# Three-stage attention and mixer kernel: ScalarE moves both accumulator halves, and the orders of the seam, the tail terms and the last sums change

## The chip, the cores and the metric

The kernel runs on one core of a Trainium2 chip. The core has engines with queues of their own: TensorE (PE in the profile, its weight loads PEld), VectorE (DVE), ScalarE (ACT), GpSimd (POOL) and SyncE (SP, which here only issues DMAs). Each engine executes its instructions in the order in which they were written; engines wait for one another through semaphores. The metric is the device time of one execution in microseconds (us), lower is better.

## The reference

Three blocks follow one another: attention with pooled queries, a gated block with spatial mixing, and a token and channel mixer. All tensors are float32.

```python
q_pool = q.reshape(B, H, S // 2, 2, D).mean(axis=3)            # B 4, H 8, S 1152, D 64
scores = 1.0 / np.sqrt(D) * np.matmul(q_pool, k.transpose(0, 1, 3, 2))
attn = softmax(scores)                                          # 576 x 1152 for each head
x = heads_side_by_side(np.matmul(attn, v))                      # [4, 576, 512]

h = gelu_tanh(x @ w_in)                                         # [4, 576, 1024]
u, v = h[..., :512], h[..., 512:]
v_n = (v - mean(v)) / np.sqrt(var(v) + 1e-06) * g_ln
v_s = np.einsum('ts,bsd->btd', w_sg, v_n) + b_sg[None, :, None]
x = x + (u * v_s) @ w_out

h = np.maximum(x.transpose(0, 2, 1) @ w_tok1, 0.0) @ w_tok2     # 576 -> 256 -> 576
u = x + h.transpose(0, 2, 1)
out = u + np.maximum(u @ w_ch1, 0.0) @ w_ch2                    # 512 -> 1536 -> 512
```

## The kernel before

Every float32 product outside the value products and transposes is made of three: each operand is split into a rounded high part and a low rest (high by ScalarE or GpSimd, low by VectorE or GpSimd), and `three` (L785) issues high x high, low x high and high x low. `stacked` (L791) does with two products for the fifth token tile, which has 64 rows: its high and low parts lie one above the other in `n_tail` and `xn_tail`, those of two batches in one pair of tiles, even batch and odd batch.

The activations stay in SBUF as `xT` [128, 16 slabs, 576], transposed; a slab is a pair of heads, four slabs are a batch.

Attention runs over 16 pairs of heads i, each in 9 steps s (four query tiles of the first head, one tile with the last 64 queries of both heads at `TAIL_STEP` 4, four tiles of the second head). In a step TensorE transposes the probabilities of four steps ago (`transpose_p`, L661), multiplies some of the transposed probabilities of the pair before with v (`values`, L732, in the bank `ACC_BANK`, first half of the queries on partitions 0 to 63, second half on 64 to 127), and makes scores in banks 0 to 3 (`scores`, L698). VectorE takes the scores out with their maximum (`take`, L1247), ScalarE does the exponential (`exps`, L1043), VectorE the reciprocal of the sum (`recip`, L1258), GpSimd the scaling (`norm`, L570), and ScalarE and VectorE move half of the transposed probabilities each (`evac_p`). The value products of a pair's first head end in step 3 of the next pair, those of its second head in step 8; then the accumulator is moved to `xT`: the first 288 queries by ScalarE (`acc_copy`, L1057), the other 288 by VectorE (`acc_copy`, L1271). The first `values` of the next head waits for both. Step 8 has its value products first, the other steps the transposes. The order on each engine is written out by `step` (L750, L1062, L1276).

The seam comes next. TensorE makes the first two v tiles of batch 0 (`v_tile`, L800) between the value products, then the rest of the value products, then `gated` (L884), which follows the list `GELU`: for batch 0 u 0, v 2, v 3, v 4, u 1, u 2, u 3. v tile 2 uses the bank of v tile 0 and waits for its gelu. A gelu takes a square and a tanh of ScalarE (L1097, L1108) and two operations of VectorE (`poly`, L1322, and `gelu`, L1331), which for a v tile is followed by its statistics; GpSimd raises the variance to -1/2 (`norm_rstd`, L630), VectorE normalises, and the result is split into `n_h` and `n_l` or `n_tail`. The orders at the seam stand in L1154 to L1172 for ScalarE and in L1433 to L1451 for VectorE; `sg_hi` and `sg_lo` split w_sg, `xe_hi_of` and `xe_lo_of` split the tails of x for v tile 4. GpSimd splits w_out behind its wait for the last accumulator copy (L625), and SP loads b_row and g_col behind the same (L503).

The spatial products are pairs of banks e = 4 to 7 (`pair`, L841), with five terms for each of two halves of the tokens, one half after the other; for e = 4 the fifth term waits for `n_tail`.

In the last block `to_tokens` (L820) transposes x, `h1_product` (L921) makes the first token product, in which batch b uses its rows of `xn_tail`; `tokens_lo` (L1376) fills both halves of it and signals once. `token_mix` (L945) makes four u products in banks 4 to 7, and VectorE adds each to `xT` (`u_added`). In the last batch VectorE does four subtractions (`u_lo_of(0)`) ahead of these four sums. Then come four chunks of 512 tokens and one of the four tails (`chunk`, L1017), all five with f products in banks 0 to 3 and y products in banks 4 to 7.

## Time and profile before

| | us |
|---|---|
| median of 3 runs | 1028.44 (1027.86 to 1028.56) |
| the profiled execution | 1028.56 |
| its span, first to last instruction | 1026.8 |
| TensorE busy | 992.4 |
| VectorE busy | 585.4 |
| ScalarE busy | 446.2 |
| GpSimd busy | 382.3 |

The first v tile starts at 440.6 us of the span, the tokens of the last block at 652, the chunks at 727. The granted TensorE clock is 0.995 of the full one in the mean. Matmul ends in the profile are modelled and overlap the next start, so steps are best read from start to start. In a timeline a number in brackets is the idle time of that engine before the row, with what ended it; rows of one kind that follow closely are merged, with their count.

### The profile page before, as it was taken

To read this page: it belongs to the slowest core of one execution; us is meant where nothing else is said; L and a number is where in the kernel's file an instruction comes from. 1 tells how busy PE (TensorE), PEld (TensorE's weight loads), DVE (VectorE), ACT (ScalarE), POOL (GpSimd) and SP (SyncE) were. 2 spreads that over 40 slices of the span, in tenths; PEclk is the share of its full clock that TensorE was granted. 3 is DMA by queue.
4 is the path that set the end of the run, shared out by engine and by line. 5 is a ranking of instruction groups with operands and counts; after the bars stand their busy time and mean duration, and the time that the engine had idled before them with its cause. 6 is when DMAs were issued, how large, how long until landed. Compare 5 with 4: busy or idle time off the path is not lost.

```text
span 1026.8 us, 23142 instructions
## 1 busy us (share of the span) xinstructions
PE 992.4 (97%) x8980; PEld 816.3 (80%) x8980; DVE 585.4 (57%) x1157; ACT 446.2 (43%) x846; POOL 382.3 (37%) x296
## 2 busy tenths in 40 slices
PE   7799999999999999889999999999999999999998
PEld 7577777777777767659999999988888888888898
DVE  5687877777778887778585867554312113131121
ACT  3677777777777777645151523131111111011111
POOL 3777777777777777631000102287000000000000
PEclk9999999999999999999999999999999999999999
DMA  5644444444444433320000000143000001001010
GB/s 164 183 117 116 115 115 115 115 115 115 115 115 115 115 89 78 112 79 1 1 2 1 2 1 1 55 115 102 1 1 15 26 0 41 0 0 41 0 41 22
DMA packets 34026, 65.54 MB, mean 64 GB/s; under 512 B 6208, under 2 KB 14784, under 8 KB 33984
## 3 DMA queue, kind: packets, MB, share of 16 engines
q1 hardware_dynamic: 33824, 64.34, 22.1%
q10 hardware_dynamic: 160, 0.59, 0.2%
q8 instruction: 32, 0.52, 0.2%
q14 instruction: 10, 0.08, 0.0%
HBM read 42.93 MB, written 4.72 MB: 46 GB/s over the span
## 4 chain that ended last, share of the span: by engine, by line
PE 83%; DVE 7%; issue 5%; DMA 2%; POOL 1%; ACT 1%; SPq 0%; DVEq 0%; ACTq 0%; POOLq 0%
PE ps L787 17%; PE ps L788 16%; PE ps L789 16%; PE ps L745 12%; PE ps L728 10%; PE ps L679 6%; DVE prob L1254 2%; PE ps L714 1%; DVE pT L1269 1%; PE ps L715 1%; PE ps L716 1%; PE ps L836 1%; DMA q_two<-in_q 1%; POOL prob L575 1%; DVE gbuf L1326 1%
## 5 line engine op out<-in xcount | busy, mean ns | idle before, releaser
L1254 DVE TENSOR_SCALAR_CACHE_REDUCE prob<-ps 128x1152 f32<-128x1152 f32 x144 | 195.5, 1358 | 74.2 <-PE ps L728 55.8
L575 POOL TENSOR_SCALAR prob<-prob,rsum 128x1152 f32<-128x1152 f32 x144 | 177.6, 1233 | 114.4 <-DVE rsum L1263 114.0
L1047 ACT ACTIVATE prob<-prob,nmax 128x1152 f32<-128x1152 f32 x144 | 181.1, 1258 | 16.8 <-DVE prob L1254 10.0
L745 PE MATMUL ps<-pT,v_sb 128*64 128x288 f32 x1152 | 171.5, 420 | 2.0
L1493 DVE SCALAR_TENSOR_TENSOR f_l<-ps,f_h 128x512 fp32r<-128x512 f32 (+1 forms) x60 | 38.3, 638 | 222.7 <-ACT f_h L1204 222.7
L1034 ACT ACTIVATE pT<-ps 128x512 f32<-128x512 f32 (+1 forms) x288 | 109.5, 432 | 97.6 <-PE ps L679 97.5
L1204 ACT ACTIVATE f_h<-ps 128x512 fp32r<-128x512 f32 (+1 forms) x60 | 33.3, 555 | 256.3 <-PE ps L789 256.3
L728 PE MATMUL ps<-k_over,q_over 64*128 64x288 f32 x744 | 131.2, 309 | 4.0 <-DVE prob L1254 4.0
L728 PEld LDWEIGHTS ps<-k_over,q_over 64*128 64x128 f32 x744 | 102.4, 185 | 24.2 <-DVE prob L1254 22.7
L679 PEld LDWEIGHTS ps<-ident,prob 64*128 64x128 f32 x2592 | 99.6, 139 | 20.4 <-issue 20.4
L679 PE MATMUL ps<-ident,prob 64*128 64x64 f32 x2592 | 106.9, 224 | 6.1 <-POOL prob L575 3.0
L745 PEld LDWEIGHTS ps<-pT,v_sb 128*64 128x64 f32 x1152 | 71.2, 136 | 44.1 <-issue 8.7
L1269 DVE COPY pT<-ps 128x512 f32<-128x512 f32 x144 | 98.9, 687 | 10.0 <-PE ps L679 10.0
L788 PE MATMUL ps<-u_l,c_h 128*128 128x512 f32 (+1 forms) x240 | 88.3, 368 | 0.0
L787 PE MATMUL ps<-u_h,c_h 128*128 128x512 f32 (+1 forms) x240 | 88.3, 368 | 0.0
L789 PE MATMUL ps<-u_h,c_l 128*128 128x512 f32 (+1 forms) x240 | 88.3, 368 | 0.0
L787 PE MATMUL ps<-f_h,c_h 128*128 128x512 f32 (+1 forms) x240 | 88.3, 368 | 0.0
L788 PE MATMUL ps<-f_l,c_h 128*128 128x512 f32 (+1 forms) x240 | 88.3, 368 | 0.0
L789 PE MATMUL ps<-f_h,c_l 128*128 128x512 f32 (+1 forms) x240 | 88.3, 368 | 0.0
L728 PE MATMUL ps<-kh,qh 64*128 64x288 f32 x248 | 85.1, 343 | 2.1 <-DMA k_over<-kl 2.1
L634 POOL TENSOR_TENSOR rstd<-var_e,minus_half 128x1 f32<-128x1 f32 x18 | 13.7, 761 | 162.5 <-DVE var_e L1351 162.5
L728 PE MATMUL ps<-kl,qh 64*128 64x288 f32 x248 | 72.4, 292 | 0.0
(153 smaller groups left out, 2144.0 us busy)
## 6 DMA issues: line engine op xcount, KB each, us to landing
q_raw<-in_q SPq DMA_DIRECT2D x16, 640.0 KB, 4.9
k_raw<-in_k SPq DMA_DIRECT2D x16, 576.0 KB, 3.9
v_sb<-in_v SPq DMA_DIRECT2D x32, 288.0 KB, 2.9
k_over<-kh SPq DMA_DIRECT2D x31, 144.0 KB, 2.5
k_over<-kl SPq DMA_DIRECT2D x31, 144.0 KB, 2.6
out_x<-xT SPq DMA_DIRECT2D x4, 1024.0 KB, 4.2
q_over<-qh SPq DMA_DIRECT2D x31, 128.0 KB, 2.3
q_over<-ql SPq DMA_DIRECT2D x31, 128.0 KB, 2.4
```

Of the source, the lines that this page charges most:

```text
L575: g.tensor_scalar(sl, sl, rsum[:, s:s + 1], 0.0, ALU.mult, ALU.add).then_inc(norm_done, 1)
L679: ins = te.transpose(dst, prob[half, PROB_BUF[s], j * P:(j + 1) * P], ident[half, half])
L728: ins = te.matmul(ps[:, 2 * m + t, 0:CK], w, x, start=(term == 0), stop=(term == 2))
L745: ins = te.matmul(ps[PH * c:PH * c + PH, ACC_BANK, 0:n], v_sb[:, a, j, :], pT[:, a, j, c * n:c * n + n], start=(j == 0), stop=(j == KB - 1))
L787: te.matmul(acc, wh, xh, start=start, stop=False)
L788: te.matmul(acc, wh, xl, start=False, stop=False)
L789: return te.matmul(acc, wl, xh, start=False, stop=stop)
L1034: return sc.activation(o, i_, ACT.Copy)
L1047: sc.activation(sl, sl, ACT.Exp, scale=-1.0, bias=nmax[:, s:s + 1], accum_out=esum[:, s:s + 1]).then_inc(exp_done, 1)
L1254: ve.tensor_scalar(prob[:, PROB_BUF[s], :].rearrange("p (c n) -> p c n", c=SCORE_BANKS), ps[:, 0:SCORE_BANKS, 0:CK], -SCALE, BIG, ALU.mult ...
L1269: ve.tensor_copy(pT_of(s, 1), trans(1)).then_inc(pT_by_dve, 1)
L1493: ve.scalar_tensor_tensor(out=f_l[:, f % F_N, 0:n], in0=ps[:, f % F_N, 0:n], scalar=0.0, in1=f_h[:, f % F_N, 0:n].bitcast(F32), op0=ALU.ma ...
```

## The change

In attention ScalarE moves both halves of the accumulator in two instructions, and VectorE moves none; one semaphore, `acc_moved`, counts four for a pair. At the seam tanh and gelu of v tiles 0 and 1 move ahead of the last accumulator copy, w_sg's last subtraction and the x tails behind it, and GpSimd's first two `norm_rstd` ahead of the w_out split. For e = 4 the fifth terms of both halves follow the first four terms of both. The odd half of `xn_tail` gets a semaphore of its own, `xn_odd`. In the last batch the u products use banks 4, 6, 0 and 2, VectorE does two of the four subtractions ahead of the first sum and two ahead of the fourth, and the first chunk is written out of the loop with waits for the sums.

```diff
@@ -376,6 +376,11 @@
+        def u_bank(b, c):
+            return (4, 6, 0, 2)[c] if b == B - 1 else 4 + 2 * (c % 2)
@@ -500,8 +505,7 @@
-            sp.wait_ge(acc_by_act, 2 * NP)
-            sp.wait_ge(acc_by_dve, 2 * NP)
+            sp.wait_ge(acc_moved, 4 * NP)
             sp.dma_start(b_row[:, :], b_sg.partition_broadcast(P)).then_inc(small_in, 16)
@@ -622,19 +626,21 @@
-            pool.wait_ge(acc_by_act, 2 * NP)
-            pool.wait_ge(acc_by_dve, 2 * NP)
-            for u in range(U_WO, U_T1):
-                split_w(u)
+            norm_rstd(0, 0)
+            norm_rstd(0, 1)
+            pool.wait_ge(acc_moved, 4 * NP)
+            for u in range(U_WO, U_T1):
+                split_w(u)
             for b in range(B):
-                for m in range(tiles(b)):
+                for m in range(2 if b == 0 else 0, tiles(b)):
                     norm_rstd(b, m)
@@ -733,8 +739,7 @@
                     if not (isinstance(i, int) and i + a == 0):
-                        pe.wait_ge(acc_by_act, at(i, 2, a))
-                        pe.wait_ge(acc_by_dve, at(i, 2, a))
+                        pe.wait_ge(acc_moved, at(i, 4, 2 * a))
                     last = TAIL_STEP if a == 0 else NS - 1
@@ -801,6 +806,9 @@
                     pe.wait_ge(xe_split, b // 2 + 1)
+                    if b == 0:
+                        pe.wait_ge(acc_moved, 4 * NP)
                     pe.wait_ge(res_done, 4 * b + RES_N - 1)
@@ -859,7 +867,19 @@
                     pe.wait_ge(sgT_lo, TT)
+                    for c in range(2):
+                        for m, (wh, wl, xh, xl) in enumerate(terms[:-1]):
+                            if c == 0:
+                                pe.wait_ge(n_ready, v_no(b, m))
+                            three(ps[:, b0 + c, 0:HALF], wh, wl, xh[:, halves[c]], xl[:, halves[c]], m == 0, False)
+                    pe.wait_ge(n_ready, v_no(b, TT - 1))
+                    for c in range(2):
+                        wh, wl, xh, xl = terms[-1]
+                        ins = stacked(ps[:, b0 + c, 0:HALF], wh, wl, xh[:, halves[c]], xl[:, halves[c]], False, True)
+                    ins.then_inc(pair_mm, 1)
+                    return
                 if e == 8 and b == B - 1:
@@ -872,8 +892,6 @@
                     for m, (wh, wl, xh, xl) in enumerate(terms):
-                        if e == 4 and c == 0:
-                            pe.wait_ge(n_ready, v_no(b, m))
                         if e == 8 and c == 0:
@@ -934,12 +951,14 @@
                         else:
+                            if o == 0 and b % 2:
+                                pe.wait_ge(xn_odd, b // 2 + 1)
                             te.matmul(ps[:, 2 + o, :], t1_h[:, t, sl], xn_tail[:, b, :], start=False, stop=False)
                         pe.wait_ge(tail_put, 2)
-                        pe.wait_ge(xn_lo, 5)
+                        pe.wait_ge(xn_odd, 1)
                         to_tokens(5)
@@ -952,12 +971,12 @@
                 for c in range(KT_N):
-                    b0 = 4 + 2 * (c % 2)
+                    b0 = u_bank(b, c)
                     sl = slice(c * P, (c + 1) * P)
-                    if c >= 2:
+                    if c >= 2 and b < B - 1:
                         pe.wait_ge(u_added, b * KT_N + ONE + c - 1)
                     if c == 0 and b == 0:
-                        pe.wait_ge(xn_lo, 6)
+                        pe.wait_ge(xn_odd, 2)
                     if c == 1 and b < B - 1:
@@ -993,6 +1012,9 @@
                 pe.wait_ge(f_free, at(c, CHT, f + 1))
+                if isinstance(c, int) and c == 0 and f < F_N:
+                    pe.wait_ge(u_added, ONE + KT_N * B - (1 if f < 2 else 0))
                 n = B * LEFT if isinstance(c, int) and c == B else CN
@@ -1021,7 +1043,8 @@
-            with pe.Fori(0, B) as c:
+            chunk(0)
+            with pe.Fori(1, B) as c:
                 chunk(c)
@@ -1057,7 +1080,9 @@
                 act.wait_ge(acc_ready, at(i, 4, 2 * a + 2))
-                copy(xT[PH * a:PH * a + PH, i, 0:HALF], ps[0:PH, ACC_BANK, 0:HALF]).then_inc(acc_by_act, 1)
+                for c in range(2):
+                    copy(xT[PH * a:PH * a + PH, i, c * HALF:(c + 1) * HALF],
+                         ps[PH * c:PH * c + PH, ACC_BANK, 0:HALF]).then_inc(acc_moved, 1)
@@ -1121,7 +1146,8 @@
                     square(b, e)
-                    tanh(b, e - 1)
+                    if (b, e) != (0, 2):
+                        tanh(b, e - 1)
                     if GELU[b][e - 2][0] == "v":
@@ -1164,12 +1190,13 @@
             sg_hi(2)
+            tanh(0, 0)
             square(0, 1)
+            sg_hi(3)
+            tanh(0, 1)
+            sg_hi(4)
             acc_copy(NP - 1, 1)
-            sg_hi(3)
-            sg_hi(4)
             xe_hi_of(0)
-            tanh(0, 0)
             for b in range(B):
@@ -1268,11 +1295,6 @@
-            def acc_copy(i, a):
-                dve.wait_ge(acc_ready, at(i, 4, 2 * a + 2))
-                ve.tensor_copy(xT[PH * a:PH * a + PH, i, HALF:SQ], ps[PH:P, ACC_BANK, 0:HALF]).then_inc(acc_by_dve, 1)
@@ -1283,8 +1305,6 @@
                     recip(i - 1, s - 2 + NS)
-                if not first and s in (TAIL_STEP - 1, NS - 1):
-                    acc_copy(i - 1, 0 if s == TAIL_STEP - 1 else 1)
                 if not tail:
@@ -1378,9 +1398,9 @@
                     ve.tensor_tensor(xn_tail[QL:P, 2 * m, :], ps[0:QL, token_bank(n), :],
-                                     xn_tail[0:QL, 2 * m, :].bitcast(F32), ALU.subtract)
+                                     xn_tail[0:QL, 2 * m, :].bitcast(F32), ALU.subtract).then_inc(xn_lo, 1)
                     ve.tensor_tensor(xn_tail[0:QL, 2 * m + 1, :], ps[QL:P, token_bank(n), :],
-                                     xn_tail[QL:P, 2 * m + 1, :].bitcast(F32), ALU.subtract).then_inc(xn_lo, 1)
+                                     xn_tail[QL:P, 2 * m + 1, :].bitcast(F32), ALU.subtract).then_inc(xn_odd, 1)
                 else:
@@ -1391,7 +1411,8 @@
                         norm_v(b, GELU[b][e - 2][1])
-                    gelu(b, e - 1)
+                    if (b, e) != (0, 2):
+                        gelu(b, e - 1)
                     if GELU[b][e - 2][0] == "v":
@@ -1442,22 +1463,27 @@
             sg_lo(2)
+            gelu(0, 0)
             poly(0, 1)
-            acc_copy(NP - 1, 1)
             sg_lo(3)
+            gelu(0, 1)
+            dve.wait_ge(acc_moved, 4 * NP)
             sg_lo(4)
             xe_lo_of(0)
-            gelu(0, 0)
             dve.wait_ge(small_in, 32)
+            def u_lo_tile(c, e):
+                dve.wait_ge(u_hi, at(c, KT_N, e + 1))
+                ve.tensor_tensor(wide(c, u_l[:, e, :]), slab_of(c, e), wide(c, u_h[:, e, :]).bitcast(F32), ALU.subtract)\
+                    .then_inc(u_split, 1)
                 for e in range(KT_N):
-                    dve.wait_ge(u_hi, at(c, KT_N, e + 1))
-                    ve.tensor_tensor(wide(c, u_l[:, e, :]), slab_of(c, e), wide(c, u_h[:, e, :]).bitcast(F32), ALU.subtract)\
-                        .then_inc(u_split, 1)
+                    u_lo_tile(c, e)
@@ -1470,11 +1496,12 @@
                         tokens_lo(n)
-                else:
-                    u_lo_of(0)
                 for f in range(KT_N):
+                    if b == B - 1 and f in (0, KT_N - 1):
+                        u_lo_tile(0, 0 if f == 0 else 2)
+                        u_lo_tile(0, 1 if f == 0 else 3)
                     dve.wait_ge(u_ready, b * KT_N + f + 1)
-                    b0 = 4 + 2 * (f % 2)
+                    b0 = u_bank(b, f)
                     x_f = slab(b, f).rearrange("p (c n) -> p c n", c=2)
```

## Rows read from the trace of the kernel before

**Rows 1.** The profile's first part: busy us (share of the span) and instructions of each engine.

```profile
PE 992.4 (97%) x8980; PEld 816.3 (80%) x8980; DVE 585.4 (57%) x1157; ACT 446.2 (43%) x846; POOL 382.3 (37%) x296
```

**Rows 2.** Timeline of TensorE, one pair of heads: start, us, engine, line, operation, tiles, count.

```profile
206.57 0.29 PE L728 MATMUL ps<-k_over,q_over 64*128 64x288 f32 x1
...
207.50 0.71 PE L745 MATMUL ps<-pT,v_sb 128*64 128x288 f32 x4
...
208.47 0.40 PE L714 MATMUL ps<-kh,qh 128*128 128x288 f32 x1 [0.26 <-DVE prob L1254]
...
212.85 0.29 PE L728 MATMUL ps<-kh,ql 64*128 64x288 f32 x1
...
222.10 1.68 PE L745 MATMUL ps<-pT,v_sb 128*64 128x288 f32 x12
```

**Rows 3.** Timeline of VectorE, same pair.

```profile
206.55 0.46 DVE L1274 COPY xT<-ps 64x288 f32 x1
207.05 1.36 DVE L1254 TENSOR_SCALAR_CACHE_REDUCE prob<-ps 128x1152 f32<-128x1152 f32 x1
...
213.21 1.36 DVE L1254 TENSOR_SCALAR_CACHE_REDUCE prob<-ps 128x1152 f32<-128x1152 f32 x1 [0.62 <-PE ps L728]
...
221.38 0.46 DVE L1274 COPY xT<-ps 64x288 f32 x1
```

**Rows 4.** Timeline of ScalarE, same pair.

```profile
206.04 0.40 ACT L1034 ACTIVATE xT<-ps 64x288 f32 x1 [0.45 <-PE ps L745]
206.35 1.24 ACT L1047 ACTIVATE prob<-prob,nmax 128x1152 f32<-128x1152 f32 x1
...
221.17 0.40 ACT L1034 ACTIVATE xT<-ps 64x288 f32 x1
...
225.40 0.77 ACT L1034 ACTIVATE pT<-ps 128x512 f32<-128x512 f32 x2 [0.57 <-PE ps L679]
```

**Rows 5.** Timeline of TensorE, end of attention.

```profile
436.89 0.78 PE L679 MATMUL ps<-ident,prob 64*128 64x64 f32 x18 [0.16 <-ACT pT L1034]
```

**Rows 6.** Timeline of TensorE, the seam.

```profile
454.00 0.29 PE L789 MATMUL ps<-x_h,wi_l 128*128 128x288 f32 x1
458.32 0.80 PE L787 MATMUL ps<-wi_h,x_h 128*128 128x512 f32 x1 [4.03 <-DVE v_f L1345]
...
466.71 0.39 PE L787 MATMUL ps<-wi_h,xe_h 128*128 128x512 f32 x1
...
469.46 0.29 PE L787 MATMUL ps<-x_h,wi_h 128*128 128x288 f32 x1
```

**Rows 7.** Timeline of VectorE, the seam.

```profile
441.83 1.42 DVE L1312 TENSOR_TENSOR sg_l<-sg_raw,sg_h 128x576 fp32r<-128x576 f32 x2
...
452.13 3.97 DVE L1312 TENSOR_TENSOR sg_l<-sg_raw,sg_h 128x576 fp32r<-128x576 f32 x2 [0.69 <-ACT sg_h L1034]
```

**Rows 8.** Timeline of GpSimd, the seam.

```profile
452.74 2.74 POOL L583 TENSOR_TENSOR wo_l<-stage,wo_h 128x1024 fp32r<-128x1024 f32 x1
```

**Rows 9.** Windows: stretch, us, busy of PE, PEld, DVE, ACT, POOL, clock, DMA, GB/s.

```profile
460.00:462.00 2.00, 2.00 (x6) 1.52 (x6) 1.72 (x4) 0.63 (x1) 0.29 (x1) 0.50 0.25 66
```

**Rows 10.** Timeline of TensorE, first spatial product of batch 0.

```profile
480.44 0.29 PE L789 MATMUL ps<-sg_h,n_l 128*128 128x288 f32 x1
481.12 0.40 PE L793 MATMUL ps<-sg_h,n_tail 128*128 128x288 f32 x1 [0.38 <-DVE n_tail L1365]
```

**Rows 11.** Timeline of TensorE, first token product.

```profile
670.30 0.39 PE L789 MATMUL ps<-xn_h,t_l 128*128 128x512 f32 x1
671.07 0.50 PE L937 MATMUL ps<-xn_tail,t_h 128*128 128x512 f32 x1 [0.38 <-DVE xn_tail L1382]
```

**Rows 12.** Timeline of VectorE, odd half of the token tail.

```profile
670.32 0.69 DVE L1382 TENSOR_TENSOR xn_tail<-ps,xn_tail 64x512 fp32r<-64x512 f32 x1
```

**Rows 13.** Timeline of TensorE, u products of the last batch.

```profile
722.47 0.29 PE L789 MATMUL ps<-t_h,h_l 128*128 128x288 f32 x1
723.99 0.40 PE L787 MATMUL ps<-t_h,h_h 128*128 128x288 f32 x1 [1.23 <-DVE xT L1479]
```

More of the change, by code:

```diff
@@ L241, in build @@
         acc_ready = sem("acc_ready")
-        acc_by_act = sem("acc_by_act")
-        acc_by_dve = sem("acc_by_dve")
+        acc_moved = sem("acc_moved")
         sgT_hi = sem("sgT_hi")
@@ L274, in build @@
         xn_lo = sem("xn_lo")
+        xn_odd = sem("xn_odd")
         h1_ready = sem("h1_ready")
```

## The prediction, made before the changed kernel was built or timed

> **What bounds the kernel now.** I read the page first. TensorE is busy 97% of the span, the next engine 57% [rows 1]. So time comes off only where TensorE stands still or runs slowly, and a row of another engine counts only if TensorE waits for it. Then I read TensorE's own timeline for its gaps, beside the timelines of VectorE and ScalarE at the same places, and last the granted clock by windows. Ends of products are modelled, so I measure a gap from start to start and subtract the undisturbed step: 0.13 us for 288 columns, 0.23 us for 512. A first product after a wait is shown with 0.40 us against 0.29 us, so a stop costs another 0.11 us [rows 2].
>
> **The change part by part.** Five parts, each read from its own stage.
>
> *Accumulator copies.* Each pair of heads has two moves of the accumulator, and each is now 0.40 us on ScalarE beside 0.46 us on VectorE [rows 3, 4]. VectorE's 32 copies go, ScalarE gets 32.
> - First head (step 3). The last score product of that step starts at 206.57, and VectorE's next take of scores at 207.05 [rows 2, 3]. Undisturbed, a take follows the last product after 213.21 - 212.85 = 0.36 us, so it would start at 206.93. The copy holds it up by 0.12 us, and TensorE then waits for that take until 208.47 [rows 2]. Nothing else is as late: the four records of the value product that come before start at 207.50 and take 0.14 us each, so they are through at 208.06. The pattern repeats with 0.10 to 0.12 us in 14 pairs and is absent in the last loop one: 14 x 0.11 = 1.5 us gained.
> - Second head (step 8). VectorE's copy delays the take there by 0.6 us too, but TensorE is busy with twelve value records from 222.10 to about 223.7 [rows 2], and the take would end well before: worth nothing.
> - ScalarE's new copy. The exponential behind the first copy starts 206.35 - 206.04 = 0.31 us later, so instructions overlap and the second copy costs 0.31 us of queue [rows 4]. Queued behind it are an exponential, a transposed-probability copy and another exponential; ScalarE then waits 0.57 us for TensorE at 225.40 [rows 4], which covers it. The value product at 222.10 waits for the moved accumulator: before, VectorE's copy ended at 221.38 + 0.46 = 221.84; now ScalarE's second ends at 221.17 + 0.31 + 0.40 = 221.88. Against that TensorE has one wait fewer. I take zero; the bounds are a gain of 0.5 us and a loss of 15 x 0.1 = 1.5 us.
> - At the end of attention the cover is missing: TensorE waits at 436.89 for a ScalarE copy [rows 5], in a chain of ScalarE instructions that the second copy of step 8 heads. Loss 0.31 us.
>
> The Trainium skill (ScalarE: Activation LUTs, What ACT_TABLE_LOAD costs) gives 186 ns plus 0.833 ns an element for an activation with immediate scale, and an overlap of 93 ns back to back: an estimate of 0.43 us for 288 elements, 0.33 us of queue. The rows' 0.40 and 0.31 us are near; by the page the copy would end 0.05 us later, 0.7 us in all over 15 pairs. The same page (Rules for kernel authors) sends plain operations to VectorE rather than ScalarE, which speaks against this edit; for this tile the trace differs, 0.46 us on VectorE against 0.40 us.
>
> *Seam.* TensorE's last product of u tile 0 starts at 454.00, and the next (v tile 2) at 458.32, when VectorE's first gelu product releases it [rows 6]. That tile was finished long before; its tanh stood in ScalarE's queue behind the last copy, and its gelu in VectorE's behind the last copy, two subtractions for w_sg (3.97 us, overlapping GpSimd's weight split) and one for x's tails [rows 7, 8]. Now tanh and gelu of v tiles 0 and 1 stand ahead of the last copy. Between v tile 1 and v tile 2 TensorE has 36 value records (36 x 0.14 = 5.0 us) and u tile 0 (24 x 0.13 = 3.2 us): 8.2 us, in which VectorE has to do about ten instructions of some 0.7 us, as 1.42 us for two shows [rows 7]. So v tile 2 follows at 454.13, a gap of 4.19 us gone. The standing still also costs clock: in 460 to 462 the granted clock is 0.50, the lower of the two levels, 1.2 GHz [rows 9], and 24 products take 466.71 - 458.32 = 8.39 us where 12 at the full 2.4 GHz take 469.46 - 466.71 = 2.75 us [rows 6]. That is 8.39 - 5.50 = 2.89 us. Together 7.1 us. Next late is v tile 4, which needs w_sg's last subtraction not at all and the x-tail subtraction at 459.6; these now start at about 451.8 behind the moved accumulator. At the slowed rate of the rows (2.0 and 1.5 us) they end at 455.4, 4 us early. GpSimd's two roots move ahead of its wait for the same copy, where it had nothing to do, so they cost nothing and the weight split starts as before, 0.3 us later. SP's loads of b_row and g_col, and the weight loads behind them, also start 0.3 us later; VectorE asks for them after 455, as they land.
>
> The Trainium skill (SBUF — State Buffer, Who interferes with whom) says that a VectorE instruction with two SBUF inputs and a GpSimd one that reads SBUF lock each other out for a whole instruction. The trace agrees: 2.0 us a subtraction, against 0.7 when GpSimd is silent [rows 7]. With one full GpSimd split (2.74 us, [rows 8]) ahead of each subtraction the pair would end near 458.7, still ahead of 459.6.
>
> *Tail terms.* In the first spatial product of batch 0 the tail term starts at 481.12, its forerunner at 480.44 [rows 10]: 0.68 - 0.13 + 0.11 = 0.66 us lost on VectorE's n_tail. The new order puts the second half's 12 products (1.6 us) in between. Batch 2 has the same gap, batches 1 and 3 need no new tail: 2 x 0.66 = 1.3 us.
>
> *Tokens.* The first tail product waits until 671.07, its forerunner starts at 670.30 [rows 11]: 0.77 - 0.23 + 0.11 = 0.65 us. It needs the even half alone, which is complete when the odd one's subtraction starts at 670.32 [rows 12], before TensorE is through at 670.53. The odd half ends at 671.0, and the transposes that need it come at 671.0. Gain 0.6 us.
>
> *Last sums.* TensorE stops at 722.60 and starts again at 723.99 [rows 13] for banks 4 and 5, which VectorE's first sum had to free behind four subtractions: 1.52 - 0.13 + 0.11 = 1.50 us. With banks 0 to 3 two more u products run at once, until 725.8. The new wait ahead of the first f product asks for the third sum, which ends about 725.1; its fourth operand at about 726.4 is needed at 727.9, and the fourth sum (727.1) by the third f product at 731. Gain 1.5 us. Writing the first chunk out of its loop I cost at nothing.
>
> **Sum**, against the profiled execution of 1028.56 us (span 1026.8 us): 1.5 - 0.3 + 7.1 + 1.3 + 0.6 + 1.5 = 11.7 us, so 1016.9 us. That execution stands 0.12 us over the median of 1028.44 us.
>
> **The rivals.**
> - *VectorE's backlog takes some of the seam back.* From the end of v tile 4 (469.46) VectorE needs 11.66 us until n_tail lets TensorE go at 481.12 [rows 6, 10]; TensorE's own way there is three u tiles (9.6 us) and, in the new order, 3.2 us of spatial products: 12.8 us, so 1.1 us of cover. Now VectorE starts this with the late w_sg subtraction, the x tails and three n subtractions under GpSimd's split. Three of them slowed by 1.25 us give 3.8 us, less 1.1: 2.7 us back, 1019.6 us. Against it: gelu(0,1), 1.8 us of its work, is done beforehand.
> - *ScalarE becomes late in the loop.* If copy, signal and wait put the value product of step 0 off by 0.25 us in 15 pairs, 3.8 us go: 1020.7 us. For it: only 0.1 us or so separates 221.88 from the point at which TensorE gets there. Against it: VectorE's copy ended at nearly the same time.
> - *The seam's edit doesn't do what it says*, since TensorE then stands in v tile 4 on the moved accumulator or the x tails: only 1 of 7 us is gained, 1023 us.
> - *Slower.* The second copy reads partitions 64 to 127, which ScalarE's copies never did here. If that form took long, it would put off the value product of step 0 in each of 15 pairs, us for us. All 11.7 us are gone when it takes 1.2 us instead of 0.40; at 1.4 us the kernel takes 1031.5 us. Against it: VectorE's copy of that form takes 0.46 us [rows 3], and ScalarE's copies that go crosswise, from the low partitions to the high, take the same as the straight ones [rows 4].
>
> **How the numbers follow.** Forecast 0.67 (its own range 1015.3 to 1018.3 us), backlog 0.15, late ScalarE 0.12, seam without effect 0.03, slower 0.03. The predicted time is the forecast's. Leaving out no more than 2 in 10 and taking in the bounds of the unknown waits gives 1015.2 to 1020.0 us. About 0.2% (2.1 us) is what a measurement can tell from no change; only the slower case and mixtures of the others end near or above: faster 0.94, same 0.03, slower 0.03.
>
> **What would show it.** After the change TensorE has no gap of over 0.3 us between u tile 0 and v tile 2, and the granted clock stays at 1.00 through 470. The pair of heads takes about 25.84 us instead of 25.95. The product after the take of step 3 starts 0.11 us sooner. The tail terms, the first token tail and the third u product follow without a wait. ScalarE's second copy is 0.40 us long and adds 0.31 us. The prediction is wrong if value products start later against the transposes before them, if TensorE waits for a gelu or an n tile after 459, or if the clock falls anywhere in the seam.

## The result and the profile after

The changed kernel takes 1015.69 us (median, 1014.56 to 1016.55) against 1028.15 us for the kernel before beside it; the ratio is 0.9885 with a 95% interval of 0.9861 to 0.9909. The forecast was 1016.9 us. The profiled execution of the changed kernel took 1014.56 us, its span is 1012.8 us: 14.0 us less than in the profile of before. The first part of its page, busy us, share of the span and instructions of each engine:

```profile
PE 988.7 (98%) x8980; PEld 814.9 (80%) x8980; DVE 570.0 (56%) x1125; ACT 460.9 (46%) x878; POOL 382.3 (38%) x296
```

Against [rows 1] 32 instructions left VectorE (15.4 us) and 32 came to ScalarE (14.7 us). TensorE's busy time fell by 3.7 us though it does the same work; v tiles 2 and 3 alone, which ran partly at the lower clock before, account for about 2.9 us of it.

Where the 14.0 us lie, read from the starts of the same instructions in both timelines (a take is VectorE's first pass over a step's scores; pairs are counted from 0):

| stage | before | after | gained |
|---|---|---|---|
| start to the first take of pair 2 | 69.08 | 68.03 | 1.05 |
| pairs 2 to 14 | 338.08 | 336.30 | 1.78 |
| pair 15 to the first v tile, without the next row | 30.97 | 31.32 | -0.35 |
| pair 15: what lies between the third take and the fourth beyond the same distance in the loop (the wait for w_in) | 2.51 | 1.17 | 1.34 |
| first product of u tile 0 to v tile 2 | 7.48 | 3.29 | 4.19 |
| v tile 2 to u tile 1 | 11.14 | 8.21 | 2.93 |
| u tile 1 to the first w_out product of batch 0 (the tail term of batch 0) | 30.50 | 30.16 | 0.34 |
| batch 2: first spatial product to batch 3's v tile 0 | 15.56 | 14.85 | 0.71 |
| first token product to the first u product | 9.40 | 8.99 | 0.41 |
| first u product to the last | 49.77 | 48.24 | 1.53 |

All other stages agree within 0.05 us. The rows of after that answer to those of before follow, in timelines with the columns of front: start, us, engine, line, operation, tiles, count, idle time before with its releaser.

One pair of heads. TensorE:

```profile
204.75 0.29 PE L734 MATMUL ps<-k_over,q_over 64*128 64x288 f32 x1
...
206.53 0.40 PE L720 MATMUL ps<-kh,qh 128*128 128x288 f32 x1
...
219.34 0.78 PE L685 MATMUL ps<-ident,prob 64*128 64x64 f32 x18
220.18 1.68 PE L750 MATMUL ps<-pT,v_sb 128*64 128x288 f32 x12
```

VectorE:

```profile
205.11 1.36 DVE L1281 TENSOR_SCALAR_CACHE_REDUCE prob<-ps 128x1152 f32<-128x1152 f32 x1 [0.44 <-PE ps L734]
```

ScalarE:

```profile
204.21 0.84 ACT L1057 ACTIVATE xT<-ps 64x288 f32 x2 [0.45 <-PE ps L750]
204.95 1.24 ACT L1070 ACTIVATE prob<-prob,nmax 128x1152 f32<-128x1152 f32 x1
...
219.22 0.83 ACT L1057 ACTIVATE xT<-ps 64x288 f32 x2
220.07 1.26 ACT L1070 ACTIVATE prob<-prob,nmax 128x1152 f32<-128x1152 f32 x1
```

The take of step 3 starts 0.36 us after the last product (204.75 to 205.11), where it took 0.48 us in [rows 2, 3], and TensorE's next scores start without the wait of 0.26 us. The two copies take 0.84 us, and the exponential follows them by 0.74 us (204.21 to 204.95) where one copy took 0.31 us [rows 4]. The value products of step 0 start 0.84 us after their transposes (219.34 to 220.18).

The seam, TensorE's first products of v tiles 2 and 3, the tail tile and u tile 1, and two windows (stretch, us, busy of PE, PEld, DVE, ACT, POOL, clock, DMA, GB/s):

```profile
450.31 0.39 PE L792 MATMUL ps<-wi_h,x_h 128*128 128x512 f32 x1
...
453.06 0.39 PE L792 MATMUL ps<-wi_h,x_h 128*128 128x512 f32 x1
...
455.78 0.39 PE L792 MATMUL ps<-wi_h,xe_h 128*128 128x512 f32 x1
...
458.52 0.29 PE L792 MATMUL ps<-x_h,wi_h 128*128 128x288 f32 x1
```

```profile
450.00:452.00 2.00, 2.00 (x12) 1.71 (x11) 0.64 (x2) 0.65 (x1) 2.00 (x1) 1.00 0.35 55
...
454.00:456.00 2.00, 2.00 (x10) 1.66 (x9) 2.00 (x3) 0.55 (x1) 2.00 (x1) 1.00 0.67 230
```

Every tile follows the last in 2.72 to 2.75 us, none waits, and the granted clock is 1.00 in both windows, where it was 0.50 in [rows 9].

The tail term of batch 0, the end of the first token product, and the third u product of the last batch:

```profile
471.10 0.29 PE L794 MATMUL ps<-sg_h,n_l 128*128 128x288 f32 x1
471.44 0.40 PE L798 MATMUL ps<-sg_h,n_tail 128*128 128x288 f32 x1
...
658.49 0.40 PE L956 MATMUL ps<-xn_tail,t_h 128*128 128x512 f32 x1
658.72 0.40 PE L957 MATMUL ps<-xn_tail,t_l 128*128 128x512 f32 x1
659.14 0.63 PE L833 MATMUL ps<-ident,x_tail 128*128 128x128 f32 x4
...
709.98 0.30 PE L794 MATMUL ps<-t_h,h_l 128*128 128x288 f32 x1
710.11 0.29 PE L792 MATMUL ps<-t_h,h_h 128*128 128x288 f32 x1
```

Two small stops are left. Between 471.10 and 471.44 TensorE has to wait for n_tail, 0.34 us where 0.13 us is the undisturbed step. Between 658.72 and 659.14 it waits for the odd half of the token tail, 0.42 us where 0.23 us is undisturbed. The third u product stands in an unbroken row.

### The profile page after: what moved, and what is told of

Same layout as the page of the kernel before. It is cut to its first block, busy times and chain, and to the rows that moved or that the text cites. A ratio compares the mean times of both kernels' runs of the same rounds, so it can differ in the third digit from the quotient of the medians.

```text
span 1012.8 us, 23079 instructions
## 1 busy us (share of the span) xinstructions
PE 988.7 (98%) x8980; PEld 814.9 (80%) x8980; DVE 570.0 (56%) x1125; ACT 460.9 (46%) x878; POOL 382.3 (38%) x296
## 4 chain that ended last, share of the span: by engine, by line
PE 91%; DVE 3%; issue 2%; POOL 1%; DMA 1%; ACT 1%; SPq 0%; DVEq 0%; ACTq 0%; POOLq 0%
PE ps L792 18%; PE ps L793 18%; PE ps L794 18%; PE ps L750 14%; PE ps L734 11%; PE ps L685 7%; DVE prob L1281 2%; PE ps L720 1%; PE ps L722 1%; PE ps L721 1%; DMA q_two<-in_q 1%; PE ps L844 1%; POOL prob L579 1%; PE ps L798 0%; PE ps L799 0%
## 5 line engine op out<-in xcount | busy, mean ns | idle before, releaser
L1281 DVE TENSOR_SCALAR_CACHE_REDUCE prob<-ps 128x1152 f32<-128x1152 f32 x144 | 195.5, 1357 | 84.0 <-PE ps L734 66.4
L734 PE MATMUL ps<-kh,ql 64*128 64x288 f32 x248 | 72.6, 293 | 0.0
```

Source lines behind the costliest of these rows:

```text
L734: ins = te.matmul(ps[:, 2 * m + t, 0:CK], w, x, start=(term == 0), stop=(term == 2))
L1281: ve.tensor_scalar(prob[:, PROB_BUF[s], :].rearrange("p (c n) -> p c n", c=SCORE_BANKS), ps[:, 0:SCORE_BANKS, 0:CK], -SCALE, BIG, ALU.mult ...
```

## The experiments

Times are medians. The kernel before ran beside them again, with medians of 1027.24, 1026.91 and 1027.85 us. Executions of one kernel differ by up to 6 us, while stages of two profiles in which nothing was changed, no DMA is awaited and the clock doesn't fall agree within 0.1 us; so most verdicts rest on a stage beside the median. The edits are shown in excerpt: lines of the same edit on other engines are left out.

**The copies alone, in the kernel before.** The kernel before with `acc_copy` of ScalarE in two instructions, VectorE's left out, one semaphore:

```diff
+                for c in range(2):
+                    copy(xT[PH * a:PH * a + PH, i, c * HALF:(c + 1) * HALF],
+                         ps[PH * c:PH * c + PH, ACC_BANK, 0:HALF]).then_inc(acc_moved, 1)
-                ve.tensor_copy(xT[PH * a:PH * a + PH, i, HALF:SQ], ps[PH:P, ACC_BANK, 0:HALF]).then_inc(acc_by_dve, 1)
```

> The kernel before with the accumulator edit alone: ScalarE moves both halves, VectorE none; every other order is that of before. Theory A (the edit is worth only the take of step 3 that no longer waits for VectorE's copy; what the changed kernel gained beyond that in attention, 1.05 us at the start and 2.05 us in the last pair, comes and goes between runs): 14 pairs x 0.14 us less 0.3 to 1.06 us at the end of attention, 0.9 to 1.6 us faster, about 1027 us; the pair of heads takes 25.82 us instead of 25.95. Theory B (the whole surplus in attention is the edit's own work): 3.8 us faster, about 1024.5 us, and the trace shows the same short start and short last pair as the changed kernel's.

1025.59 us, ratio 0.9987 (0.9976 to 0.9998): 1.3 us faster by the ratio, theory A. Pairs 2 to 11 take 258.18 us, 25.82 us each.

**The change without the copies.** The changed kernel with the copies shared again, both signalling on `acc_moved`:

```diff
-                for c in range(2):
+                for c in range(1):
                     copy(xT[PH * a:PH * a + PH, i, c * HALF:(c + 1) * HALF],
+                ve.tensor_copy(xT[PH * a:PH * a + PH, i, HALF:SQ], ps[PH:P, ACC_BANK, 0:HALF]).then_inc(acc_moved, 1)
```

> The changed kernel with the accumulator shared in attention as before: ScalarE moves the first half of the queries, VectorE the second, at the same places of their queues as in the kernel before, the last one at the seam included. Theory A: 0.9 to 1.6 us slower than the changed kernel, about 1016.8 us, the pair of heads back at 25.95 us, and the loss of 1.06 us at the end of attention gone. Theory B: 3.8 us slower, about 1019 us.

1015.74 us, no difference from the changed kernel. Neither theory's time came. The pair takes 25.86 us (258.55 for ten), not 25.95, though VectorE copies as in the kernel before, and the delay of 0.11 us ahead of the take of step 3 is back. So 0.10 us a pair came from something else that the change brought: the one semaphore.

**One semaphore alone.**

```diff
-                        pe.wait_ge(acc_by_act, at(i, 2, a))
-                        pe.wait_ge(acc_by_dve, at(i, 2, a))
+                        pe.wait_ge(acc_moved, at(i, 4, 2 * a))
```

> The kernel before with one edit: both accumulator copies stay where they are, but both signal on one semaphore, and TensorE's first value product of a head has one wait in place of two. Theory D (each wait of TensorE that comes last costs about 0.1 us, so that a part of what the change gained in the loop is the semaphore's and not the copy's): the pair of heads takes 25.85 us instead of 25.95, the value product of step 0 starts 0.71 us after its transposes instead of 0.82, 1.4 us faster in all. Rival (the semaphores are worth nothing; the pair varies so much between runs): 25.95 us and no difference in time.

1024.45 us against 1026.91, ratio 0.9977 (0.9966 to 0.9989). The pair takes 25.86 us. TensorE's transposes of step 0 in the kernel before, and with one semaphore the same transposes and the value products behind them:

```profile
221.28 0.78 PE L679 MATMUL ps<-ident,prob 64*128 64x64 f32 x18
```

```profile
219.64 0.77 PE L676 MATMUL ps<-ident,prob 64*128 64x64 f32 x18
220.38 1.68 PE L741 MATMUL ps<-pT,v_sb 128*64 128x288 f32 x12
```

What was 0.82 us (221.28 to the 222.10 of [rows 2]) became 0.74 us. Theory D holds for the pair. The median fell by more (2.5 us) than 14 x 0.10 us; the interval reaches from 1.1 to 3.5 us and holds both.

**Only the first head by ScalarE.** The changed kernel with the second head's copies shared:

```diff
-                for c in range(2):
+                for c in range(2 - a):
                     copy(xT[PH * a:PH * a + PH, i, c * HALF:(c + 1) * HALF],
```

> The changed kernel, but only for the first head of each pair does ScalarE move both halves; those of the second head (step 8, and the last one at the seam) are shared as before. Theory A (the second head's edit gains nothing, and its second ScalarE copy delays the chain at the end of attention): the pair of heads stays at 25.82 us, the 1.06 us at the end of attention come back; 0.3 to 1.1 us faster than the changed kernel, about 1014.8 us. Rival (the second head's edit is worth something in the loop): the pair of heads is longer than 25.85 us and the time is that of the changed kernel or above.

1015.26 us. The medians don't tell it from the changed kernel, the profile does: the pair takes 25.74 us against 25.81, and the value products follow their transposes by 0.71 us.

```profile
218.67 0.77 PE L685 MATMUL ps<-ident,prob 64*128 64x64 f32 x18
219.38 1.68 PE L750 MATMUL ps<-pT,v_sb 128*64 128x288 f32 x12
```

So theory A was too mild: the second head's copy on ScalarE doesn't gain nothing, it costs 0.08 us a pair. My expectation also held a misreading. The "1.06 us at the end of attention" was counted from the ninth take of pair 15, and that take had moved: without VectorE's copy ahead of it, it starts 0.6 us earlier. From the first take of pair 15 to the first v tile, less the wait for w_in, it is 30.97 us before, 31.32 us after, 30.76 us here. The end of attention costs the change 0.35 us, and the second head's part alone 0.56 us.

**VectorE moves both halves.**

```diff
+                for c in range(2):
+                    ve.tensor_copy(xT[PH * a:PH * a + PH, i, c * HALF:(c + 1) * HALF],
+                                   ps[PH * c:PH * c + PH, ACC_BANK, 0:HALF]).then_inc(acc_moved, 1)
```

> The changed kernel turned round: VectorE moves both halves, ScalarE none. This doubles what the edit took away. Theory A (the take of scores in step 3 is what TensorE waits for, and the copy's 0.46 us stands ahead of it): the take starts 0.12 + 0.46 = 0.58 us later than in the changed kernel, 14 x 0.58 = 8.1 us, less about 1 us that comes back at the end of attention; about 1022 us, the pair of heads 26.4 us. The copies ahead of the take of step 8 cost nothing. Rival (another wait takes over, or VectorE catches up): under 3 us slower than the changed kernel, the pair of heads under 26.0 us.

1027.79 us, 12 us slower than the changed kernel; the pair takes 26.70 us. VectorE's takes and copies at steps 3 and 8:

```profile
207.28 1.36 DVE L1278 TENSOR_SCALAR_CACHE_REDUCE prob<-ps 128x1152 f32<-128x1152 f32 x1 [0.43 <-PE ps L734]
...
209.56 0.94 DVE L1299 COPY xT<-ps 64x288 f32 x2
210.53 1.36 DVE L1278 TENSOR_SCALAR_CACHE_REDUCE prob<-ps 128x1152 f32<-128x1152 f32 x1
...
222.03 1.36 DVE L1278 TENSOR_SCALAR_CACHE_REDUCE prob<-ps 128x1152 f32<-128x1152 f32 x1 [0.43 <-PE ps L734]
...
224.84 0.94 DVE L1299 COPY xT<-ps 64x288 f32 x2
225.82 1.36 DVE L1278 TENSOR_SCALAR_CACHE_REDUCE prob<-ps 128x1152 f32<-128x1152 f32 x1
```

From take to take it is 3.25 us at step 3 (210.53 - 207.28), 0.58 us over the 2.67 of the changed kernel, as worked out. The other 0.31 us of the 0.89 us a pair come at step 8, where I had said a copy ahead of the take costs nothing. With one copy there nothing shows (first head only, 25.74 us a pair); with two the cover is used up.

**A third copy on ScalarE.** The changed kernel with a further copy ahead of the second:

```diff
+                    if c and not (isinstance(i, int) and i == NP - 1 and a == 1):
+                        copy(spare[PH * a:PH * a + PH, :], ps[PH * c:PH * c + PH, ACC_BANK, 0:HALF])
```

> The changed kernel in which ScalarE makes one more copy of the same size ahead of its second accumulator copy (into a spare tile that nobody reads; left out at the seam). It makes the second copy 0.42 us later, the size at which the slower rival of the prediction decides. Theory E (the value product of step 0 has no slack left, since it already starts 0.84 us after its transposes instead of 0.71): it is put off by 0.42 us in each of 15 pairs, 6.3 us slower than the changed kernel, about 1022 us, the pair of heads 26.2 us. Rival (ScalarE's queue has slack here): under 1.5 us slower, the pair of heads under 25.9 us.

1020.28 us, 4.6 us slower than the changed kernel. ScalarE and TensorE at step 8 and 0:

```profile
222.37 0.40 ACT L1058 ACTIVATE xT<-ps 64x288 f32 x1
222.79 0.41 ACT L1058 ACTIVATE spare<-ps 64x288 f32<-64x288 f32 x1
223.10 0.39 ACT L1058 ACTIVATE xT<-ps 64x288 f32 x1
```

```profile
222.49 0.77 PE L686 MATMUL ps<-ident,prob 64*128 64x64 f32 x18
223.63 1.68 PE L751 MATMUL ps<-pT,v_sb 128*64 128x288 f32 x12 [0.37 <-ACT xT L1058]
```

The extra copy takes 0.31 us of queue, not 0.42. The value products start 1.14 us after their transposes instead of 0.84, the pair takes 26.12 us instead of 25.81: 0.30 us for 0.31 us, in 15 pairs 4.5 us. Theory E holds in its mechanism, us for us, and the size of the copy was mine to miss.

**The weights of the last pair later.**

```diff
-            body(NP - 1, 1, last=True, w0=2, w=(0, 2, 4, 6))
+            body(NP - 1, 1, last=True, w0=2, w=(1, 3, 5, 7))
```

> The changed kernel with GpSimd's four steps for the last two pieces of w_in one step later in the last pair of heads (steps 1, 3, 5 and 7 in place of 0, 2, 4 and 6). Theory C (the last pair's surplus and the spread between runs come from GpSimd, which stands 2.3 to 4.7 us on the landing of the third piece of w_in with a normalisation queued behind it that TensorE's transposes need): the first to the ninth take of the last pair takes 22.3 us instead of 23.4, as in the loop; the fastest runs 1.1 us faster and the slower ones 3 us, median about 1013.5 us with a narrower spread. Rival (the spread has another cause, and the piece would land late for the next step as well): the median stays at 1015.7 us and the last pair keeps a stall of a microsecond or more.

1013.76 us, ratio to the kernel before 0.9874 (0.9856 to 0.9893), 1.9 us below the changed kernel's first median and 1.6 us below its second (1015.33, further down). The first to the ninth take of pair 15 takes 22.24 us, as in the loop. GpSimd's wait in the changed kernel and here:

```profile
408.16 1.05 POOL L539 TENSOR_SCALAR wi_h<-stage 128x1024 fp32r<-128x1024 f32 x1 [2.33 <-DMA stage<-in_moe_w_in]
```

```profile
409.14 1.05 POOL L539 TENSOR_SCALAR wi_h<-stage 128x1024 fp32r<-128x1024 f32 x1 [1.94 <-DMA stage<-in_moe_w_in]
```

GpSimd still waits 1.94 us, but the normalisation is ahead of the wait now and TensorE waits for nothing. In the changed kernel TensorE waits behind it:

```profile
410.56 0.77 PE L685 MATMUL ps<-ident,prob 64*128 64x64 f32 x18 [0.96 <-POOL prob L579]
```

**Gelu of v tile 1 late.**

```diff
             sg_lo(3)
-            gelu(0, 1)
```

> The changed kernel with tanh and gelu of v tile 1 back in the list behind the last accumulator copy, where the kernel before has them; those of v tile 0 stay ahead of it. It gives VectorE 1.8 us more of work behind the copy, the backlog of the prediction's first rival. Theory F (VectorE is late there by now): v tile 3 waits for this gelu by about 0.6 us, and the wait for n_tail in the first spatial product grows from 0.2 us to about 2.0 us; about 2.4 us slower than the changed kernel, 1018 us. Rival (the backlog is absorbed before the first spatial product): only the wait of v tile 3, or none, under 0.7 us slower.

1017.04 us, 1.4 us slower by the median; from the first v tile to the last product 2.5 us (574.55 against 572.04), near the 2.4 us expected, at three places:

```profile
452.81 0.50 PE L792 MATMUL ps<-wi_h,x_h 128*128 128x512 f32 x1 [0.33 <-DVE v_f L1363]
...
467.63 0.41 PE L792 MATMUL ps<-x_h,wi_h 128*128 128x288 f32 x1 [1.13 <-DVE v_f L1363]
...
473.21 0.40 PE L798 MATMUL ps<-sg_h,n_tail 128*128 128x288 f32 x1 [0.54 <-DVE n_tail L1383]
```

The first cost 0.61 us. The second, 1.40 us, I had overlooked: the second half of u tile 3 waits for the gelu of v tile 4. The third cost 0.49 us more than in the changed kernel, not 1.8, since that wait took the backlog first. VectorE has no room to spare here: without the gelu ahead of the copy nearly the first rival's 2.7 us are lost.

**The last sums: VectorE's order alone, the banks alone.**

```diff
-            return (4, 6, 0, 2)[c] if b == B - 1 else 4 + 2 * (c % 2)
+            return 4 + 2 * (c % 2)
```

> The changed kernel with half of the last sums' edit: VectorE's order is the new one (two subtractions ahead of the first sum, two ahead of the fourth), but the last batch's u products use banks 4 and 6 in turn and wait for the sums as before. By the times of the changed kernel the first sum ends at 710.27 us, and the third u product would start at 709.94: a stop of 0.33 + 0.11 = 0.4 us. Theory G (the stop of before was VectorE's order, the banks only take away its rest): the stage from the first u product of the changed kernel's last block to its last (48.24 us there, 49.77 before) takes 48.7 us. Rival (the banks are what counts): about 49.7 us.

The stage took 48.61 us, theory G (the profiled execution 1018.54 us). TensorE at the third u product:

```profile
713.62 0.29 PE L794 MATMUL ps<-t_h,h_l 128*128 128x288 f32 x1
713.97 0.40 PE L792 MATMUL ps<-t_h,h_h 128*128 128x288 f32 x1
```

```diff
+                if b == B - 1:
+                    u_lo_of(0)
                 for f in range(KT_N):
-                    if b == B - 1 and f in (0, KT_N - 1):
-                        u_lo_tile(0, 0 if f == 0 else 2)
-                        u_lo_tile(0, 1 if f == 0 else 3)
```

> The changed kernel with the other half of the last sums' edit: banks 4, 6, 0 and 2, but VectorE makes all four subtractions ahead of the first sum, as before. The third sum then ends about 712.9 us and the first f product asks for it at 713.3; the fourth ends at 714.3, asked for at 717. Theory G': no stop at the third u product and none at the first f product, the stage takes 48.24 us as in the changed kernel and the chunks start 0.41 us behind it: the order on VectorE was not needed beside the banks. Rival (the prediction's reason for the order: the sums come late and the first f product waits): the chunks start 0.5 to 1.3 us later than in the changed kernel.

48.28 us, and the chunks start 0.40 us behind the last u product: theory G' (1018.42 us). VectorE makes all four subtractions first, and TensorE doesn't wait:

```profile
712.14 2.49 DVE L1481 TENSOR_TENSOR u_l<-xT,u_h 128x512 fp32r<-128x512 f32 x4
714.55 2.08 DVE L1505 TENSOR_TENSOR xT<-ps,xT 128x576 f32<-128x576 f32 x3
717.35 0.76 DVE L1505 TENSOR_TENSOR xT<-ps,xT 128x576 f32<-128x576 f32 x1 [0.73 <-PE ps L794]
```

**The changed kernel again.**

> The changed kernel itself once more, for a second profile and more times on the chip on which the combined kernel runs. If what varies in it is the start of attention and the last pair of heads alone, its stages from the second to the twelfth pair (258.14 us) and from the first v tile on (572.04 us to the last product) come out the same within 0.1 us, and only the first two pairs and the last one differ, by up to 3 us together.

1015.33 us (1014.43 to 1016.83), ratio 0.9877 (0.9859 to 0.9895). Pairs 2 to 11 took 258.20 us, from the first v tile to the last product 572.09 us. The first take of pair 2 came at 67.17 us (68.03 in the other profile), and the wait for w_in in pair 15 cost 2.7 us (1.17). GpSimd in this execution:

```profile
408.84 1.04 POOL L539 TENSOR_SCALAR wi_h<-stage 128x1024 fp32r<-128x1024 f32 x1 [3.85 <-DMA stage<-in_moe_w_in]
```

**What the runs point to, together.** First head by ScalarE, second shared, the last pair's weights later, and GpSimd's first piece one step earlier:

```diff
-            body(NP - 3, 1, w0=0, w=(7, 8))
+            body(NP - 3, 1, w0=0, w=(6, 7))
-            body(NP - 1, 1, last=True, w0=2, w=(0, 2, 4, 6))
+            body(NP - 1, 1, last=True, w0=2, w=(1, 3, 5, 7))
```

> What the runs so far point to: the changed kernel with ScalarE moving both halves for the first head only and the copies of the second head shared (1.1 us in the loop, 1.1 us at the end of attention), the last pair's weight pieces in steps 1, 3, 5 and 7 (1.1 us, and up to 3 in slow landings), and GpSimd's first piece in steps 6 and 7 instead of 7 and 8 of its pair, since its subtraction holds up a normalisation of the next pair (0.8 us). If these add up: 4.1 us below the changed kernel of the same call, about 1011 us. If the gains share one slack: under 3 us below it.

1010.89 us (1009.42 to 1010.96), ratio to the kernel before 0.9827 (0.9813 to 0.9842), 4.4 us below the changed kernel of the same group (1015.33), where 4.1 us was expected: the gains add up. Pair 14 lost its surplus of 0.8 us (25.71 us against 26.50), pair 15 has none. TensorE is busy 98% of a span of 1009.1 us:

```profile
PE 990.0 (98%) x8980; PEld 817.4 (81%) x8980; DVE 576.4 (57%) x1141; ACT 452.6 (45%) x862; POOL 381.5 (38%) x296
```

## Why the prediction was right

The time was right, and so was the order of the terms; two of them were composed otherwise than I said. That the sum is so close is partly luck: attention gave 0.2 us more than forecast, the tail terms about 0.3 and the tokens 0.2 us less, and the largest term rests on a stretch of slow clock that is shorter in other executions.

| pairs 2 to 11, us for ten | semaphores of TensorE's wait | first head | second head |
|---|---|---|---|
| 259.55, kernel before | two | shared | shared |
| 258.56, one semaphore alone; 258.55, the change without the copies | one | shared | shared |
| 257.38, first head only | one | ScalarE | shared |
| 258.14, changed kernel; 258.20 again; 258.18, copies alone | one | ScalarE | ScalarE |
| 267.00, VectorE both | one | VectorE | VectorE |
| 261.15, third copy | one | ScalarE, three | ScalarE, three |

- *First head, 0.11 us a pair.* Right: 258.55 - 257.38 gives 0.12 us.
- *ScalarE's new copy, taken as zero.* Right as a sum and wrong as a reason. Two prices cancel: one wait of TensorE fewer gains 0.10 us a pair, the copy of the second head costs 0.08. I had named both and given neither a size. By the total of attention (1.78 - 0.35 = 1.43 us against the forecast of 1.2) it can't be seen; only the kernels with one of them tell them apart. The copies themselves are worth little: the changed kernel without them, with the one semaphore kept, takes the same time.
- *Queue of the second copy, 0.31 us.* Wrong: 0.42 us. I took the distance from a copy to the exponential behind it for that from copy to copy.
- *End of attention, -0.31 us.* Near as a sum, -0.35 us, and too small for its reason: the second head's copy, which the prediction blames, costs 0.56 us there (31.32 against 30.76), and the rest of the change gives 0.21 us back (30.97 against 30.76).
- *Seam, 7.1 us.* Right in both terms, 4.19 and 2.93 us. But the second is that of one execution. In the two other profiles with the old order TensorE stood still as long (4.21 and 3.96 us, against the 4.03 of [rows 6]), and v tiles 2 and 3 took 7.20 and 6.96 us against 8.39, which is 1.7 and 1.5 us of slow clock instead of 2.9. In the kernel with the copies alone the windows read:

```profile
455.00:457.00 2.00, 1.54 (x4) 1.29 (x5) 1.90 (x5) 0.00 (x0) 2.00 (x1) 0.70 0.53 186
457.00:459.00 2.00, 2.00 (x6) 1.52 (x5) 1.59 (x4) 0.63 (x1) 0.56 (x2) 0.50 0.20 66
459.00:461.00 2.00, 2.00 (x9) 1.60 (x9) 1.66 (x5) 0.89 (x2) 0.93 (x1) 0.95 0.00 0
```

  The clock falls to the lower level after the same stop, but for 3.4 us by these windows, where it stood at 0.50 from 457.5 to 464.3 in the profile of before. A saving of slow clock needs more than one profile.
- *Tail terms, 2 x 0.66 us.* Batch 2 gave 0.71, batch 0 only 0.34: VectorE's backlog, the first rival, at an eighth of its price. It was named, and the forecast had not taken any of it. A step of the prediction that failed feeds it: "VectorE asks for them after 455, as they land", of the loads of b_row and g_col. VectorE was through with the x tails at 450.25 and stood until g_col landed, about 0.4 us longer than ScalarE's square of u tile 0 (done at 451.16) would have kept it:

```profile
451.61 0.75 DVE L1346 SCALAR_TENSOR_TENSOR gbuf<-gbuf,ps 128x576 f32<-128x576 f32 x1 [1.36 <-DMA g_col<-in_moe_g_ln]
```

  That is more than the stop ahead of n_tail (0.21 us, 0.32 with its restart). Whether the stop goes when the loads come earlier, no run tests.
- *Tokens, 0.6 us.* 0.41 us. The step that failed is "the transposes that need it come at 671.0": they come 0.19 us before the odd half's signal, and that wait was not in the sum.
- *Last sums, 1.5 us.* Right, 1.53, but the order of VectorE, with which I worked out the new waits, was not needed beside the banks (each half of the edit in one profile); alone it gives 1.2 of the 1.5 us.
- *The rest of the 14.0 us between the two profiles.* The start (1.05 us) and the wait for w_in (1.34 us) are not the change's. With the same code up to there, six profiles have the first take of pair 2 at 66.4 to 68.9 us, and the wait for w_in costs 1.2 to 4.0 us in five. In the two with the earliest take (66.4 and 67.2 us) the granted clock is 1.00 from 8 to 60 us; in the other four it falls there for a time. Without these two the stages give 11.6 us; the sum was 11.7 us.
- *The slower rival.* Its sum was off by 0.4 us (at 1.4 us a copy, 15 x 1.0 us over 1016.9 are 1031.9). Its mechanism is real: past the point that the changed kernel has reached, each 0.31 us on ScalarE ahead of the second head's signal put the loop off by 0.30 us a pair. Only the form that reads partitions 64 to 127 was not slow: 0.40 us.
- *ScalarE late in the loop, at 0.25 us a pair,* came with 0.13 us in the value products' start (0.84 against 0.71 us) and 0.08 us in the pair.
- *The signs of being wrong.* Two of the three that the prediction named came, each small: the value products of step 0 start 0.84 us after their transposes where it was 0.82 before, and TensorE waits for an n tile after 459, 0.21 us at 471.44. The third, a fall of the clock in the seam, didn't come.

## What to carry to other kernels

A "zero" in a sum may be two terms that cancel; an experiment that does one half of an edit shows them, and here the half was better than the whole. Where an edit merges two semaphores or drops a wait on the busiest engine, price that for itself. Measure each stage from a landmark that the edit doesn't move, and read a stage with a DMA wait or a clock drop from several executions before its size goes into a sum.

## What I had not expected of the hardware

- A second semaphore to wait for ahead of a value product cost TensorE 0.10 us a pair (25.955 us with two, 25.86 with one), though both signals it asks for come about together. Why, no run here shows.
- Two 64x288 copies of ScalarE follow each other by 0.42 us where the first reads partitions 0 to 63 and the second 64 to 127, so they don't overlap; two of the latter kind follow by 0.31 us (222.79 to 223.10). The Trainium skill (ScalarE: Activation LUTs, What ACT_TABLE_LOAD costs) states that activations back to back overlap by about 93 ns; the trace agrees for the second distance, not for the first. Why the first is longer no run here shows.
- At the seam VectorE's normalisation of one tile took 2.03 us beside GpSimd's subtraction for the weights, against 0.54 us where GpSimd was idle, though it reads one large tile of SBUF. The first row is GpSimd's:

```profile
453.82 2.72 POOL L587 TENSOR_TENSOR wo_l<-stage,wo_h 128x1024 fp32r<-128x1024 f32 x1
...
454.80 2.03 DVE L1377 TENSOR_SCALAR v_f<-v_f,mv,rstd 128x512 f32<-128x512 f32 x1
...
464.67 0.54 DVE L1377 TENSOR_SCALAR v_f<-v_f,mv,rstd 128x512 f32<-128x512 f32 x1
```

  The rival of the backlog had counted the subtractions alone. The Trainium skill (SBUF — State Buffer, Who interferes with whom) says that such an operation can take the shared ports too; the trace agrees.
- The same DMA (the third piece of w_in) kept GpSimd waiting 1.5 to 4.7 us in the profiles of this case, with up to 4.0 us for TensorE behind it. Part of that is clock: with VectorE's order alone the granted clock was 0.50 from 413.0 to 416.2 us, behind this wait. It was a large part of the spread that the copies' effect had to be read through.
